# Two routed expert layers behind an attention block: layer two's down projection with the relu block as the stationary operand

## The reference, cut to what matters

```python
for e in range(E):
    mask = expert_idx == e
    h = np.maximum(x[mask] @ w1[e], 0.0)
    out[mask] = gate_w[mask, None] * (h @ w2[e])
```

## Time and profile before

| | |
|---|---|
| median of 3 runs | 1140.99 us (1136.89 to 1141.04) |
| span of the profiled execution | 1142.4 us |
| PE busy | 1074.0 us, 94% |
| DVE busy | 789.5 us, 69% |
| ACT busy | 724.2 us, 63% |
| POOL busy | 160.9 us, 14% |
| transfers, share of 16 engines | 14.3% |

### The profile page before, as it was taken

One profiled execution on the slowest core, in us unless ns is written; L12 is line 12 of the kernel. 1 busy time (PEld: TensorE's weight loads), 2 busy tenths in 40 slices (PEclk: granted clock), 3 DMA queues, 4 the chain that ended last, 5 costly groups with the idle time before them and its releaser, 6 DMA issues.

```text
span 1142.4 us, 29623 instructions
## 1 busy us (share of the span) xinstructions
PE 1074.0 (94%) x6715; PEld 610.7 (53%) x6715; DVE 789.5 (69%) x2342; ACT 724.2 (63%) x1761; POOL 160.9 (14%) x424
## 2 busy tenths in 40 slices
PE   6988876889999999999999999999999999999887
PEld 6987533445555555555555555555555555555443
DVE  4568884557776767777676777767677776767654
ACT  3458663456666666666666766666676666667553
POOL 3100001111111111111111111111111111111100
PEclk9989996889999999999999999999999999999999
DMA  8305650000000000000000000000000000000000
GB/s 332 120 22 163 212 174 21 12 21 27 27 27 27 27 26 20 26 27 27 27 27 27 19 27 27 27 27 27 27 20 26 27 27 27 27 27 18 12 22 20
DMA packets 38288, 52.89 MB, mean 46 GB/s; under 512 B 7504, under 2 KB 24056, under 8 KB 37604
## 3 DMA queue, kind: packets, MB, share of 16 engines
q1 hardware_dynamic: 38244, 52.35, 14.3%
HBM read 40.57 MB, written 11.78 MB: 46 GB/s over the span
## 4 chain that ended last, share of the span: by engine, by line
PE 91%; issue 3%; DVE 2%; ACT 1%; POOL 1%; DMA 1%; ACTq 0%; POOLq 0%; DVEq 0%
PE y L1196 41%; PE up L1219 22%; PE up L1209 7%; PE SM L1273 4%; PE TB L1116 3%; PE y L1092 2%; PE up L1084 2%; PE y L1288 2%; PE TB L1264 2%; PE up L1135 1%; PE TB L1243 1%; PE SM L1255 1%; PE up L1092 1%; PE TB L1231 1%; DMA stage<-in_moe_w 1%
## 5 line engine op out<-in xcount | busy, mean ns | idle before, releaser
L802 DVE SCALAR_TENSOR_TENSOR R<-up,R 128x500 f16<-128x500 f32 x736 | 491.0, 673 | 216.3 <-ACT R L552 216.2
L552 ACT ACTIVATE R<-up 128x500 f16<-128x500 f32 x736 | 416.1, 586 | 146.7 <-PE up L1209 79.1
L1219 PE MATMUL up<-R,W1B 128*128 (+1 forms) x1104 | 277.7, 382 | 21.1 <-issue 15.9
L1196 PE MATMUL y<-R 128*128 128x500 f16 x1104 | 292.1, 373 | 0.4 <-DVE R L802 0.4
L1196 PE MATMUL y<-R,W2A 128*128 128x500 f16 x1104 | 279.5, 375 | 1.3 <-DVE R L802 1.3
L1219 PEld LDWEIGHTS up<-R,W1B 128*128 x1104 | 108.8, 99 | 158.4 <-issue 49.5
L1196 PEld LDWEIGHTS y<-R,W2A 128*128 x1104 | 104.5, 101 | 101.1 <-issue 15.9
L1196 PEld LDWEIGHTS y<-R 128*128 x1104 | 100.3, 97 | 88.3 <-issue 3.1
L1209 PE MATMUL up<-R 128*128 (+1 forms) x368 | 138.3, 379 | 0.0
L485 POOL TENSOR_TENSOR st<-ss,root 125x4 f32<-125x4 f32 x46 | 46.8, 1018 | 386.0 <-ACT TB L584 386.0
L458 POOL CAST E<-ex 125x256 f16<-125x256 f32 x46 | 18.3, 397 | 403.7 <-ACT ex L603 403.7
(11 more groups left out here) (149 smaller groups left out, 1136.1 us busy)
## 6 DMA issues: line engine op xcount, KB each, us to landing
stage<-in_moe_w SPq DMA_DIRECT2D x24, 512.0 KB, 3.9
xin<-in_x SPq DMA_DIRECT2D x46, 250.0 KB
out<-SALL SPq DMA_DIRECT2D x46, 250.0 KB
R<-in_x SPq DMA_DIRECT2D x4, 2304.0 KB, 17.5
SALL<-in_moe_w SPq DMA_DIRECT2D x8, 512.0 KB, 4.3
R<-in_x SPq DMA_DIRECT2D x1, 2240.0 KB, 29.6
modi<-in_moe_modality_id SPq DMA_DIRECT2D x46, 3.9 KB
R<-in_x SPq DMA_DIRECT2D x1, 64.0 KB, 29.1
```

What stands on the lines that cost most here:

```text
L552: nc.scalar.activation(hhi[:, (u % UP) * CT:(u % UP + 1) * CT], ups[u % UP][:, 0:CT], ACT.Relu).then_inc(s["hi_done"], 1)
L802: nc.vector.scalar_tensor_tensor(hlo[:, o:o + CT], ups[u % UP][:, 0:CT], 0.0, hhi[:, o:o + CT], ALU.max, ALU.subtract).then_inc(s["lo_done ...
L1196: ins = mm(y[:, 0:CT], W[:, bass.ds(woff + (fb * 2 * C + o), C)], h[:, k * CT:(k + 1) * CT], start=opens and fb == 0 and n == 0, stop=fb = ...
L1219: ins = mm(ups[k][:, 0:CT], W1B[:, bass.ds(woff + (wl * F + fb * P), P)], ytb[:, bass.ds(yoff + yl * CW, CT)], start=n == 0, stop=n == 2)
```

## The change

Layer two's down projection (`down_by_point`) takes a block of 128 columns of `hhi` or `hlo` as the stationary operand and 128 columns of the weights `W2B` as the moving one. The output block then has 125 points on the partitions and 128 values in the columns, which is the form of the rows. A down part is 4 x 3 matmuls of 128 columns in place of 3 of 500. `hhi` and `hlo` get a stride of CW = 504 columns per unit in place of 500, and POOL clears them once. The copy into `yT` and the four transposes go, with their semaphores. The scaling copy into `yout` moves from behind unit 15's relu to behind unit 12's, and the constant 1 / S_OUT of the `yT` copy goes into `coef`. Layer one is unchanged.

```diff
-        hhi, hlo = (RH[:, BUF1 + k * UP * CT:BUF1 + (k + 1) * UP * CT] for k in range(2))
-        yT = RH[:, BUF1 + 2 * UP * CT:BUF1 + (2 * UP + 2) * CT].bitcast(f32)
+        hhi, hlo = (RH[:, BUF1 + k * UP * CW:BUF1 + (k + 1) * UP * CW] for k in range(2))
...
-            for m in (ytb, E4T):
+            for m in (ytb, E4T, hhi, hlo):
                 nc.gpsimd.memset(m, 0.0).then_inc(s["pads_cleared"], 1)
...
-                def yt(after):
-                    act.wait_ge(s["pass_done"], after)
-                    nc.scalar.activation(yT[:, :], y2[:, 0:CT], ACT.Copy, scale=1.0 / S_OUT).then_inc(
-                        s["result_copied"], 1)
...
-                def result():
+                def result(after):
                     act.wait_ge(s["gate_steps"], CG * (c + 3))
                     act.wait_ge(s["out_free"], c + 1)
-                    act.wait_ge(s["result_transposed"], c + 1)
+                    act.wait_ge(s["pass_done"], after)
...
-                            8: [lexps] if rx or ry else [], 10: [lambda: yt(after())] if l2 else [],
-                            13: [exps] if xq else [], 15: [result] if l2 else []}
+                            8: [lexps] if rx or ry else [], 12: [lambda: result(after())] if l2 else [],
+                            13: [exps] if xq else []}
...
-                        tell(nc.vector.tensor_tensor(coef[:, now], gs[:, 1, 1, :], c1[:, now], ALU.mult), "gate_steps")
+                        tell(nc.vector.scalar_tensor_tensor(coef[:, now], gs[:, 1, 1, :], 1.0 / S_OUT, c1[:, now], ALU.mult,
+                                                            ALU.mult), "gate_steps")
...
+                def down_by_point(woff, opens):
+                    def down(fb, k):
+                        if fb == 0 and opens:
+                            pe.wait_ge(s["result_ready"], c + 1)
+                        for j in range(TJ):
+                            for n, (h, o) in enumerate(((hhi, 0), (hhi, C), (hlo, 0))):
+                                ins = mm(y2[:, j * C:(j + 1) * C], h[:, k * CW + j * TQ:k * CW + j * TQ + P],
+                                         W2B[:, bass.ds(woff + (fb * 2 * C + o), C)],
+                                         start=opens and fb == 0 and j == 0 and n == 0, stop=fb == NF - 1 and n == 2,
+                                         skip_group_check=True)
+                        return ins
+                    return down
...
-                    return up, down_of(W2B, woff, y2, opens, before if opens else None)
+                    return up, down_by_point(woff, opens)
...
-                def out_transposes():
-                    pe.wait_ge(s["result_copied"], c + 1)
-                    for j in range(TJ):
-                        ins = nc.tensor.transpose(y2[0:TQ, j * C:(j + 1) * C], yT[:, j * TQ:(j + 1) * TQ],
-                                                  ident[:, :])
-                    ins.then_inc(s["result_transposed"], 1)
...
-                         7: when(xq, scores), 8: when(joint, counts), 12: when(l2, out_transposes)}
+                         7: when(xq, scores), 8: when(joint, counts)}
```

More of the change, by code:

```diff
@@ L89, in attention_two_moe_kernel @@
         BUF1 = BUF0 + 6 * CW
-        hhi, hlo = (RH[:, BUF1 + k * UP * CT:BUF1 + (k + 1) * UP * CT] for k in range(2))
-        yT = RH[:, BUF1 + 2 * UP * CT:BUF1 + (2 * UP + 2) * CT].bitcast(f32)
-        BUF2 = BUF1 + (2 * UP + 2) * CT
+        hhi, hlo = (RH[:, BUF1 + k * UP * CW:BUF1 + (k + 1) * UP * CW] for k in range(2))
+        BUF2 = BUF1 + 2 * UP * CW
         tmp16 = RH[:, BUF2:BUF2 + 3 * 512].rearrange("p (k n) -> p k n", k=3)
@@ L203, in attention_two_moe_kernel @@
             "flag_steps gate_steps "
-            "result_copied result_transposed result_ready out_written out_free ").split()
+            "result_ready out_written out_free ").split()
         s = {n: sem(n) for n in names}
@@ L537, in _ @@
                     nc.scalar.activation(hi, a, ACT.Copy, scale=S_W).then_inc(s["w2b_hi_ready"], 1)
-            act.wait_ge(s["pads_cleared"], 2)
+            act.wait_ge(s["pads_cleared"], 4)
             npas = act.alloc_register("act_pass")
@@ L551, in units @@
                     act.wait_ge(s["up_done"], base + (k + 1))
-                    nc.scalar.activation(hhi[:, (u % UP) * CT:(u % UP + 1) * CT], ups[u % UP][:, 0:CT],
+                    nc.scalar.activation(hhi[:, (u % UP) * CW:(u % UP) * CW + CT], ups[u % UP][:, 0:CT],
                                          ACT.Relu).then_inc(s["hi_done"], 1)
@@ L800, in units @@
                     v.wait_ge(s["hi_done"], base + (k + 1))
-                    o = (u % UP) * CT
+                    o = (u % UP) * CW
                     nc.vector.scalar_tensor_tensor(hlo[:, o:o + CT], ups[u % UP][:, 0:CT], 0.0, hhi[:, o:o + CT],
@@ L1189, in pe_step, with down_of @@
                 joint = rx or ry
-                def down_of(W, woff, y, opens, before=None):
+                def down_of(W, woff, y, opens):
                     def down(fb, k):
-                        if fb == 0 and before:
-                            before()
                         for n, (h, o) in enumerate(((hhi, 0), (hhi, C), (hlo, 0))):
-                            ins = mm(y[:, 0:CT], W[:, bass.ds(woff + (fb * 2 * C + o), C)], h[:, k * CT:(k + 1) * CT],
+                            ins = mm(y[:, 0:CT], W[:, bass.ds(woff + (fb * 2 * C + o), C)], h[:, k * CW:k * CW + CT],
                                      start=opens and fb == 0 and n == 0, stop=fb == NF - 1 and n == 2,
                                      skip_group_check=True)
+                        return ins
[10 more added lines that the diff above has]
+                                         skip_group_check=True)
                         return ins
@@ L1221, in up @@
                         return ins
-                    def before():
-                        pe.wait_ge(s["result_ready"], c + 1)
-                    return up, down_of(W2B, woff, y2, opens, before if opens else None)
+                    return up, down_by_point(woff, opens)
                 def e4():
```

## The result

The changed kernel takes 1209.8 us (median of 4 runs, 1208.7 to 1211.3) against 1138.9 us before on the same chip: a ratio of 1.06, 95% interval 1.0564 to 1.0635. It is slower, as forecast, but by 71 us where the sum gave 23; the range ended at 1175. The profiled span went from 1142.4 to 1207.2 us.

What follows compares the result with a forecast made beforehand. PE bounds the kernel, a step ending by ACT, DVE's unit 15, then PE's queue. 44 x (0.22 + 0.12) = 15.0, layer-two-only steps 0.4, end -1.5, jumps +8.8: +22.7 us, median 1164, range 1147 to 1175.

Steps and rivals of the forecast that it cites:

- Down parts: Layer two on PE: 96 matmuls of 0.055 us in place of 24 of 0.211, +0.22 us per step, bounds 0.1 to 0.4.
- Rival B: Layer two's weight loads on PE don't hide, 9.2 us per step in place of 5.06: +190 us, about 1330; chance 0.05.
- Transposes: PE at the step's end: removing their 0.43 us gains nothing in the 44 steps with both layers; bounds 0 and 0.2.
- rival A: PE's array alone bounds the step's end, so the transposes' time comes out whole: -11 us, about 1130; chance 0.05.
- ACT and DVE at the end of the step: The scaling copy behind unit 12's relu delays unit 15's remainder on DVE: +0.12 us per step, bounds 0 and 0.3.
- The signs: Trace marks of a right forecast: matmul spacing, period, PE's wait ahead of down part 14, new waits at steps 44 and 45.
- The step that failed: SP's output transfers: as many issued, the store some 3 us earlier in a step; no cost was counted.
- The -1.5: At the end of the last step, without copy and transposes, the scaling copy starts earlier: -1.5 us, once.
- The two jumps: PE's jumps over unused code at steps 44 and 45 cost 3.0 and 1.4 us each: +8.8 in all, bounds 0 and 12.
- Rival C: The loop's code no longer stays where PE's queue finds it, 4.4 us in each of 42 steps: about 1340; chance 0.04.
- A term put at nothing, in the setup: POOL's two more clearings end while ACT still converts weights: no cost, or 3.6 us once without that cover.

Runs made afterwards that it cites:

- late_store: The changed kernel, scaling copy still behind unit 12's relu, but the output transfer issued only once ACT has passed unit 15's relu; 1166.1 us, 1.0225 times the kernel before.
- before_no_transposes: The kernel before without the copy into yT and the four transposes, the scaling copy reading y2 directly, so its output is not the reference's; 1139.3 us, ratio 0.9969.
- late_copy: The changed kernel with the scaling copy behind unit 15's relu again, so the output transfer is issued at the step's end; 1167.4 us, 1.0244 times the kernel before.
- short_tail: late_store with the code for mixed chunks left out of PE's program in steps 44 and 45; 1157.4 us, 1.0125 times the kernel before.
- early_loads: The changed kernel with DVE's load of the flags behind unit 13's remainder and PE's behind unit 12's down part; 1165.4 us, 1.0217 times the kernel before.

## Why the prediction was right or wrong, point by point

**Down parts.** Forecast 0.22 us per step with a bound of 0.4; late_store's period less that of before gives 20.28 - 19.97 = 0.31. A 128-column matmul comes every 0.056 us, not 0.055, and a step holds 96 of them. Rival B, loads that don't hide, has fallen, and with it the 81 ns that the Trainium skill (TensorE: Matmul & The Clock Gate, Back-to-back issue gap) states: here twelve pairs in a row go at 0.056 us.

**Transposes.** Forecast no gain in a step with both layers; before_no_transposes shows a period of 19.98. Right, and rival A with it out.

**ACT and DVE at the end of the step.** Forecast +0.12 us from the copy behind unit 12; late_store, with the copy there, has the period of late_copy, with the copy at its old place: nothing.

**The signs.** Matmuls 0.056 us apart and new waits at steps 44 and 45 came as named. The period (21.2 us, named 20.2 to 20.5) and PE's wait ahead of down part 14 (1.17 us, named 0.5) did not; late_store, without the collision, has 20.28 and 0.21.

**The step that failed.** The prediction said: "SP issues as many; the store comes some 3 us earlier in a step", and put no price on it. It had the new time of the transfer and didn't ask what else happens in that time. The transfer takes its packets out of SBUF while DVE and PE read their flags there, the loads take 1.35 and 1.0 us in place of 0.35 and 0.33, and DVE's stands right ahead of the remainder of unit 15, the very link that the prediction had found to set the step's end. That is 21.21 - 20.28 = 0.93 us a step. PE's waits on those remainders add up to 51.5 us in the change and 10.3 in late_store, 41 us less; the medians of the two differ by 43.7, of 71 in all. The first steps differ too: at step 1 the changed kernel waits 5.09 us on "issue" and late_store 0.23, and why wasn't tested. The loads were in the trace of before, as lines of DVE's and PE's queues; the views read, of busy time, don't show them.

**The last step and the jumps.** The -1.5 came: the scaling copy starts 0.04 us after the last matmul's end in the changed kernel (1201.84) and 1.50 after it before (1137.07). The two jumps, forecast as 8.8, measured 8.7 between the medians of late_store and short_tail and 10.0 in their traces. The prediction read step 44's jump of before as costing nothing, but the trace of before has waits on "issue" of 0.62 us within step 44's first up parts and 0.87 ahead of step 45's, so against the kernel before the two come to about 8.5. Rival C didn't come: 28 instruction packets in place of 22.

**A term put at nothing, in the setup.** The prediction said of POOL's two more clearings that they end "while ACT still converts weights", at a price of 3.6 us "once if that cover were gone". ACT was covered, but DVE was not. Timeline of all engines, before and after:

```profile
125.09 2.66 POOL L449 MEMSET R<- 128x2016 f16 x2 [59.04 <-PE TB L1119]
...
127.18 0.72 DVE L766 COPY HTr<-HT 128x256 f32<-128x256 f32 x1
```
```profile
125.13 6.09 POOL L448 MEMSET R<- 128x2016 f16 x4 [58.38 <-PE TB L1114]
...
127.22 4.16 DVE L760 COPY HTr<-HT 128x256 f32<-128x256 f32 x1
```

DVE's copy into `HTr` ends 0.15 us after POOL's clearing in both, so it takes 4.16 us in place of 0.72, and PE, which waits for it, goes on 3.5 us later. late_copy, late_store and early_loads show 4.15 or 4.16. That the copy is held by the clearing is read from these ends; no run moved the clearing.

**The sum.** The starts of the first up parts divide the 64.8 us between the spans. Step 0 starts at 221.58 in place of 217.15: 4.4 us, most of it from the setup. From there step 43 is reached 52.8 us later still (1148.43 in place of 1091.18), for which 43 steps at 0.31 + 0.93 would give 53.3. The rest, from step 43 on, is 7.6 us, for which the jumps, step 43's wait and the down parts less the 1.5 would give 8.8; that 1.2 us stays open.

## What to carry to other kernels

When an edit makes a result ready earlier, its transfer starts earlier too: look at what every engine's queue does in that new slot, the register loads included, and hold the transfer back if one of them lies on the chain. Work that an engine does ahead of a wait it would have anyway is free, so find the wait before you count the saving. If a loop's period ends in "wait, then branches", try moving the wait behind the register work; here one such edit gained 1.3%. A clearing on one engine during the setup can hold another engine's copy: look there before calling it covered.

## What the runs showed of the hardware that was not expected

A register load of four words out of SBUF takes 0.31 to 0.35 us on ACT, DVE and PE, and 0.7 to 1.35 us while a transfer of 250 KB reads SBUF; a transfer of the same size that writes SBUF at 102 GB/s leaves it at 0.35. Whether it is the partition, the tile or the path that the two share was not tried. 128-column float16 matmuls, each with a weight load of its own, come every 0.056 us, twelve in a row. DVE's float32 copy of 256 columns into `HTr` took 4.16 us beside a 6.09 us clearing on POOL and 0.72 beside one of 2.66, and ended with it both times. In the steps written out, PE's jump over the unused code came with a wait of 3 to 5 us, and the matmuls behind it took 4.1 to 4.4 us in place of 2.7.
